# Folding the channel axis of a Fourier stage on Trainium2, with the first batch's Fourier part placed between the second batch's output products

## Chip, cores and metric

The kernel runs on one core of a Trainium2 chip. The metric is the device time of one execution in microseconds (us); TensorE is the matrix engine, VectorE, ScalarE and GpSimd are the elementwise engines, and SyncE issues all DMAs. In the profile they are called PE (its weight loads PEld), DVE, ACT, POOL and SP.

## What is computed

Three stages in float32, on 2 batches, 768 positions and 8 heads of 64 channels (512 channels together):

```python
# 1. attention among positions whose 6-bit hashes agree
scores = np.where(q_bucket == k_bucket, scale * q @ k.T, -1e9)
x = softmax(scores) @ v                      # (2, 768, 512)
# 2. gated projection
gate = sigmoid(causal_conv5(x, conv_w));  y = (gate * (x @ w_val)) @ w_out
# 3. Fourier mixing and a feed-forward block
mixed = np.real(np.fft.fft(np.fft.fft(y, axis=1), axis=2))
u = y + mixed
un = (u - mean(u)) / sqrt(var(u) + 1e-6)
out = u + relu(un @ w_ch1) @ w_ch2
```

## The kernel before

Every engine runs a program of its own, in the order in which it is written; semaphores tie them together. There is no scheduler: the order of calls in each engine's block is the order of work. TensorE takes float32 values that were rounded to a short form (fp32r), so nearly every operand is kept as a high and a low part, and one product (`product`, whose matmuls all carry line 1090) is three matmuls: high by high, low by high, high by low. ScalarE writes the high part, VectorE or GpSimd the low part (the value minus its high part).

- **Attention.** A software pipeline over 96 units (16 heads of 6 tiles). Before unit 0, SyncE loads the first two heads, the penalty column, then in its step -12 heads 2 and 3, the 128x128 identity (line 471), the values and the first weight chunks. VectorE converts the identity to bf16 (line 903) ahead of its first row maximum (`maximum`, line 830), since it is needed to turn the maxima.
- **Values and outputs.** `values(b, r)` forms x @ w_val for a half of a batch, in 4 banks of PSUM; VectorE multiplies it by the gate (`gate_values`, line 945), ScalarE rounds it (`hi_gv`), VectorE takes the rest (`lo_gv`, line 933). `outputs(b)` (line 1223) forms 6 tiles of y of 128 positions, each of 12 matmuls of 512 columns, and ScalarE copies them out of PSUM (`copy_y`). An output of the first 384 positions waits for the first 12 of the 16 low parts of the gated values, one of the last 384 for all 16.
- **Fourier part along the positions.** A sequence of 768 is folded: position s plus, and minus, position s+384 (`fold_tile`, line 950, 6 tiles of 128x512), which gives even and odd frequencies. `along_sequence(b)` (line 1237) has 8 groups, one for each 128 channels and parity, each of 9 matmuls with 386 or 384 columns (cosine and sine beside each other). ScalarE and VectorE split each result (`hi_seq`, `lo_seq`, lines 738 and 963).
- **Fourier part along the channels.** `along_channels(b, t)` (line 1253): for each of 6 tiles of positions, 4 blocks of 128 channels, cosine (258 columns) and sine (256), three matmuls each: 24 matmuls a tile. VectorE adds the result to y in four pieces and takes the tile's statistics (`add_mixed`, lines 972 to 980).
- **Feed-forward.** `hidden` and `project` run over 16 blocks of the hidden layer, for 4 blocks of 384 positions. Their weights are loaded through a staging buffer of two halves and split on the way: for w_1, GpSimd does chunks 0 to 9 alone (lines 529 and 597), and ScalarE (line 778) and GpSimd (line 608) share chunks 10 to 15; for w_2 GpSimd does all. ScalarE's calls alternate: two late chunks of w_1, then one tile of the turned normalised values (`hi_un`, line 751), three times; VectorE's low part of such a tile is `lo_un` (line 1020). TensorE starts `hidden(0, 0)` when all three `lo_un` are done.
- **Order.** TensorE: values and outputs of batch 0, of batch 1, then sequence and channels of batch 0, sequence and channels of batch 1, feed-forward. GpSimd: 16 chunks of the Fourier tables (`split_tables`), 6 low parts of folds (`lo_fold`, line 585), w_1 chunks 0 to 3, folds and low parts of batch 1, w_1 chunks 4 to 9, the late six, w_2.

## Time and profile before

| | before |
|---|---|
| time, median of 3 runs | 714.03 us (714.02 to 714.39) |
| time of the profiled execution | 714.04 us |
| its span, first to last instruction | 712.2 us |
| TensorE busy | 684.7 us, 96% of the span |
| VectorE, ScalarE, GpSimd busy | 388.9, 243.8, 203.0 us |
| mean granted clock of TensorE | 0.987 of full speed |
| chain that ended last | 92% TensorE, 3% VectorE, 1% DMA |

A busy share is an average over stages: the same TensorE can be without a gap in one stage and idle in the next. A row of the timeline gives the start in us from the span's start, the duration, the engine, the line, the operation, output and inputs, and in brackets how long the engine was idle before and what released it. Matmuls overlap, so the cost of one in a row of them is the distance between two starts, not its own duration.

### The profile page before, as it was taken

The numbers are of one execution on the slowest core, as the hardware profiler recorded it, in microseconds if no ns is written. First come the engines' busy times: TensorE is split into PE (matmuls) and PEld (weight loads), VectorE is DVE, ScalarE is ACT, GpSimd is POOL, SyncE is SP. The second block draws the span as 40 slices with busy tenths as digits, with TensorE's granted clock in tenths as the row PEclk, the third lists the DMA queues.
The fourth block names the chain that finished last, engine by engine and source line by source line (L and its number), as shares of the span: only waits on it lengthen the run. The fifth ranks groups of instructions, "written<-read, shape, count | busy, mean of one in ns | idle before, by whom it ended". The sixth has DMA issues, their size and how long they took to land.

```text
span 712.2 us, 10036 instructions
## 1 busy us (share of the span) xinstructions
PE 684.7 (96%) x3600; PEld 614.7 (86%) x3600; DVE 388.9 (55%) x621; ACT 243.8 (34%) x376; POOL 203.0 (29%) x193
## 2 busy tenths in 40 slices
PE   3699999999999999999999999999999999999998
PEld 2588888888888888798989999999999999999997
DVE  3566768888888888958745796321222122212112
ACT  2065545555555455654345241111112111211110
POOL 0001323232323233538848965880000000000000
PEclk9699999999999999999999999999999999999999
DMA  5945565555655441212202132330100010001001
GB/s 152 249 134 142 131 173 139 166 149 156 154 157 154 119 123 53 75 39 57 55 30 60 31 90 89 89 90 0 45 0 0 0 44 0 0 0 44 1 1 44
DMA packets 43846, 57.64 MB, mean 81 GB/s; under 512 B 21520, under 2 KB 25872, under 8 KB 43808
## 3 DMA queue, kind: packets, MB, share of 16 engines
q1 hardware_dynamic: 43808, 57.14, 29.0%
q8 instruction: 23, 0.38, 0.2%
q14 instruction: 15, 0.12, 0.1%
HBM read 31.81 MB, written 3.24 MB: 49 GB/s over the span
## 4 chain that ended last, share of the span: by engine, by line
PE 92%; DVE 3%; ACT 1%; DMA 1%; SPq 1%; issue 1%; DVEq 0%
PE psum L1090 74%; PE psum L1175 5%; PE psum L1176 4%; PE psum L1182 1%; PE psum L1183 1%; PE psum L1184 1%; PE psum L1187 1%; PE psum L1188 1%; PE psum L1185 1%; PE psum L1157 1%; DVE max_col L830 1%; PE psum L1278 1%; DMA ident<-in_ident_in 1%; DMA qk_raw<-in_qk 1%; ACT probs L669 1%
## 5 line engine op out<-in xcount | busy, mean ns | idle before, releaser
L1061 DVE SCALAR_TENSOR_TENSOR h_lo<-psum,h_hi 128x384 fp32r<-128x384 f32 x64 | 35.7, 558 | 184.2 <-ACT h_hi L791 184.2
L830 DVE TENSOR_REDUCE max_col<-psum 128x1 f32<-128x768 f32 x96 | 91.2, 953 | 40.8 <-PE psum L1090 40.6
L791 ACT ACTIVATE h_hi<-psum 128x384 fp32r<-128x384 f32 x64 | 31.5, 492 | 215.4 <-PE psum L1090 215.4
L669 ACT ACTIVATE probs<-psum 128x768 f32<-128x768 f32 x96 | 77.6, 809 | 39.8 <-PE psum L1090 39.8
L1090 PE MATMUL psum<-unt_hi,w_hi 128*128 (+1 forms) x256 | 86.9, 339 | 0.0
L1090 PE MATMUL psum<-unt_lo,w_hi 128*128 (+1 forms) x256 | 86.3, 337 | 0.0
L1090 PE MATMUL psum<-unt_hi,w_lo 128*128 (+1 forms) x256 | 85.9, 336 | 0.0
L1090 PE MATMUL psum<-a1k,a1q 128*128 128x384 f32 x192 | 67.9, 354 | 11.8 <-DVE max_col L830 6.7
L1090 PE MATMUL psum<-a1q,a1k 128*128 128x384 f32 x192 | 76.0, 396 | 0.8 <-ACT a2q L657 0.8
L1090 PE MATMUL psum<-w_lo,h_hi 128*128 128x512 f32 x192 | 75.9, 395 | 0.0
L1090 PE MATMUL psum<-w_hi,h_lo 128*128 128x512 f32 x192 | 75.8, 395 | 0.0
L1090 PE MATMUL psum<-w_hi,h_hi 128*128 128x512 f32 x192 | 74.6, 389 | 0.0
L1090 PE MATMUL psum<-a2k,a2q 96*128 96x384 f32 x192 | 67.2, 350 | 0.0
L546 POOL TENSOR_TENSOR vl<-v,vh 128x384 fp32r<-128x384 f32 x16 | 20.5, 1284 | 156.7 <-issue 81.6
L1090 PE MATMUL psum<-a2q,a2k 99*128 99x384 f32 x192 | 65.0, 339 | 0.0
L666 ACT ACTIVATE p_hi<-psum 128x768 fp32r<-128x768 f32 x48 | 39.0, 813 | 65.2 <-PE psum L1090 63.5
L836 DVE TENSOR_TENSOR p_lo<-probs,p_hi 128x768 fp32r<-128x768 f32 x48 | 54.0, 1125 | 3.2 <-ACT probs L669 3.2
L557 POOL TENSOR_TENSOR xT<-sums,rec_b 64x768 f32<-64x768 f32 x16 | 30.0, 1872 | 79.0 <-DMA rec_b<-rec_dram 74.4
L1090 PEld LDWEIGHTS psum<-unt_hi,w_hi 128*128 128x128 f32 x256 | 48.1, 188 | 2.2
L1090 PEld LDWEIGHTS psum<-unt_hi,w_lo 128*128 128x128 f32 x256 | 48.1, 188 | 2.2
L1090 PEld LDWEIGHTS psum<-a1k,a1q 128*128 128x128 f32 x192 | 38.2, 199 | 13.3 <-DVE max_col L830 7.3
L1090 PEld LDWEIGHTS psum<-unt_lo,w_hi 128*128 128x128 f32 x256 | 48.0, 188 | 0.0
(129 smaller groups left out, 1449.6 us busy)
## 6 DMA issues: line engine op xcount, KB each, us to landing
stg_w<-in_w SPq DMA_DIRECT2D x32, 256.0 KB, 2.6
qk_raw<-in_qk SPq DMA_DIRECT2D x16, 384.0 KB, 5.1
a1k<-qk_hi SPq DMA_DIRECT2D x32, 192.0 KB, 3.3
flag_b<-flag_dram SPq DMA_DIRECT2D x16, 384.0 KB, 4.2
a1q<-qk_hi SPq DMA_DIRECT2D x16, 192.0 KB, 2.8
a2q<-qk_hi SPq DMA_DIRECT2D x16, 192.0 KB, 3.5
a1q<-qk_lo SPq DMA_DIRECT2D x16, 192.0 KB, 3.7
a2k<-qk_lo SPq DMA_DIRECT2D x16, 192.0 KB, 3.7
```

The lines of the kernel that those rows point to most:

```text
L546: pool.tensor_tensor(vl[par][:, :].rearrange("p (t d) -> p t d", d=P), split_tiles(v1[par][:, :]), bits(vh[par][:, :]).rearrange("p (t d) ...
L557: pool.tensor_tensor(xT[rows, slot * S:(slot + 1) * S], sums[par][rows, :], rec_b[rows, :], ALU.mult).then_inc(x_ready, 1)
L666: act.activation(halves(p_hi[k % PHBUF][:, 0:S]), ring("st", i), ACT.Exp, scale=SCALE).then_inc(p_hi_ready, 1)
L669: act.activation(halves(probs[i % PBUF][:, 0:S]), ring("st", i), ACT.Exp, scale=SCALE).then_inc(probs_ready, 1)
L791: act.activation(h_hi[:, (j % 2) * HALF:(j % 2 + 1) * HALF], psum[:, j % 2, 0:HALF], ACT.Relu).then_inc(h_hi_ready, 1)
L830: dve.tensor_reduce(max_col[:, i % T:i % T + 1], ring("s", i), AX.XY, ALU.max).then_inc(max_done, 1)
L836: dve.tensor_tensor(p_lo[i % PBUF][:, 0:S], probs[i % PBUF][:, 0:S], bits(p_hi[k % PHBUF][:, 0:S]), ALU.subtract).then_inc(p_lo_ready, 1)
L1061: dve.scalar_tensor_tensor(h_lo[:, half], psum[:, j % 2, 0:HALF], 0.0, bits(h_hi[:, half]), ALU.max, ALU.subtract).then_inc(h_lo_ready, 1)
L1090: mm = pe.matmul(dst, lhs, rhs, start=first and n == 0, stop=last and n == len(pairs) - 1)
L1157: mm = pe.matmul(out_ps[0:MPARTS, t // HT, (t % HT) * P:(t % HT + 1) * P], neg_parts[:, MPARTS * t:MPARTS * (t + 1)], ident_b[:, :], start ...
L1175: pe.matmul(first, v1[par][:, w], probs[i % PBUF][:, 0:HALF], start=start, stop=stop)
L1176: pe.matmul(last, v1[par][:, w], probs[i % PBUF][:, HALF:PCOLS], start=start, stop=stop).then_inc(pv_done, 1)
```

## The change

- **The channel axis is folded too.** The real part of a transform over 512 channels needs channel c only together with channel 512-c: their sum meets the cosines, their difference the sines. So after the fold along the positions each tile is folded along the channels (`fold_tile`, now three VectorE instructions for one: the 512-column fold into `fold`, then a 256-column sum and a 256-column difference with the reversed half into `cf`). The sum goes only to the cosine columns and the difference only to the sine columns: `along_sequence` has 4 groups of 18 matmuls with 194 or 192 columns, and `along_channels` has 2 blocks in place of 4, 12 matmuls a tile.
- **Channel 0 has no partner.** It is carried apart: `fold_zero` (four tiny VectorE instructions), `zero_along_sequence` (12 matmuls with 2 weight columns and 194 or 192 moving ones), two small copies on ScalarE and two small subtractions on VectorE, and one more matmul a tile of `along_channels`, of 258 columns, against a row of ones. GpSimd fills that row and a tile of zeros before the tables.
- **The tables are shorter**: 16 chunks of 210 columns in place of 274.
- **The order.** Output tiles are made in the order 0, 3, 1, 4, 2, 5. TensorE does two outputs of batch 1, the whole sequence part of batch 0, then twice two tiles of its channel part and two outputs, then its last two tiles and the sequence part of batch 1. The folds of batch 0 move to VectorE's loop over the gated values of batch 1; those of batch 1 stand between the `add_mixed` of batch 0, all on VectorE. GpSimd's first four chunks of w_1 stand between its low parts of batch 1. VectorE's `inverse_deviations(0)` moves behind the split of batch 1, and the weights of the feed-forward get other addresses.
- **The identity** is loaded in SyncE's fifth DMA, and no longer in step -12.

The core of the diff:

```diff
-NE = HALF // 2 + 1
+NE = HALF // 2 + 2
 NO = HALF // 2
 EV, OD = 2 * NE, 2 * NO
+CM = CT // 2
+CH = C // 2
 NC_ = C // 2 + 2
 NS_ = C // 2
-WB_USED = HT * (EV + OD) + CT * (NC_ + NS_)
...
+WB_USED = HT * (EV + OD) + CM * (NC_ + NS_)
...
+Y_ORDER = (0, 3, 1, 4, 2, 5)
+FOLDS = (0, 3, 1, 4, 2, 5)
+NCF = 4
+SEQ = ((0, 0), (1, 0), (0, 1), (1, 1))
+SEQ_BANK = ((0, 1, 2, 3), (6, 4, 5, 7))
+ZERO_BANK = (6, 2)
+OUT_BANK = (4, 5, 7)
...
+        def channel_banks(b, t):
+            return 2 * (t % 3) if b else 2 * (t % 2)
...
             load_qk(1)
             sp.dma_start(pencol[:, :], pen_in).then_inc(pen_loaded, 16)
+            sp.dma_start(ident[:, :], ident_in).then_inc(ident_loaded, 16)
...
-                    sp.dma_start(ident[:, :], ident_in).then_inc(ident_loaded, 16)
...
+            def lo_fold(b, k):
+                n, f = T * b + k, FOLDS[k]
+                pool.wait_ge(cf_ready, 2 * (n + 1))
+                pool.wait_ge(f_hi_ready, n + 1)
+                if b > 0 and k == 0:
+                    pool.wait_ge(seq_done, len(SEQ) * b)
+                pool.tensor_tensor(f_lo[:, f * C:(f + 1) * C], cf[:, (n % NCF) * C:(n % NCF + 1) * C],
+                                   bits(f_hi[b][:, f * C:(f + 1) * C]), ALU.subtract).then_inc(f_lo_ready, 1)
...
+            pool.memset(bits(ones_row[:, :]), 1.0).then_inc(zeros_ready, 1)
+            pool.memset(bits(u0t[:, :]), 0.0).then_inc(zeros_ready, 1)
             split_tables((0, NH // 2))
-            lo_fold(0)
+            for k in range(T):
+                lo_fold(0, k)
+            pool.wait_ge(val_done, 2 * CT * B)
+            lo_fold(1, 0)
+            lo_fold(1, 1)
+            split_w1((0, W1_EARLY // 4))
+            lo_fold(1, 2)
+            lo_fold(1, 3)
+            split_w1((W1_EARLY // 4, W1_EARLY // 2))
+            lo_fold(1, 4)
+            lo_fold(1, 5)
             pool.wait_ge(y_done, B * T)
-            split_w1((0, W1_EARLY // 2))
-            fold_tile(1, 0)
-            pool.wait_ge(seq_done, 2 * CT)
-            lo_fold(1)
             split_w1((W1_EARLY // 2, (W1_N - W1_LATE) // 2))
+            pool.wait_ge(seq_done, len(SEQ) * B)
...
-            hi_gv(1)
-            for t in range(T):
-                copy_y(1, t)
-                if t < HT:
-                    hi_fold(0, 2 * t)
-                    hi_fold(0, 2 * t + 1)
-            hi_seq(0)
-            for f in range(T):
-                hi_fold(1, f)
+            for k in range(HT, T):
+                copy_y(0, k)
+            for i in range(2 * CT):
+                hi_gv(1, i)
+                if i < T:
+                    hi_fold(0, i)
+            copy_y(1, 0)
+            copy_y(1, 1)
+            hi_spectrum(0)
+            for k in range(2, T, 2):
+                hi_fold(1, k - 2)
+                hi_fold(1, k - 1)
+                copy_y(1, k)
+                copy_y(1, k + 1)
+            hi_fold(1, T - 2)
+            hi_fold(1, T - 1)
+            hi_spectrum(1)
             deviations(0)
-            hi_seq(1)
...
+            def fold_tile(b, k):
+                n, f = T * b + k, FOLDS[k]
                 kt, odd = f % HT, f // HT
+                base = n % 2 * C
+                dve.wait_ge(y_ready, T * b + 2 * (kt + 1))
+                dve.tensor_tensor(fold[:, base:base + C], y3[:, T * b + kt, :], y3[:, T * b + kt + HT, :],
+                                  ALU.subtract if odd else ALU.add).then_inc(fold_ready, 1)
+                dve.wait_ge(fold_ready, n + 1)
+                if n >= NCF:
+                    dve.wait_ge(f_lo_ready, n - NCF + 1)
+                up, down = fold[:, base + 1:base + CH + 1], fold[:, base + C - 1:base + CH - 1:-1]
+                dst = cf[:, n % NCF * C:(n % NCF + 1) * C]
+                dve.tensor_tensor(dst[:, 0:CH], up, down, ALU.add).then_inc(cf_ready, 1)
+                dve.tensor_tensor(dst[:, CH:C], up, down, ALU.subtract).then_inc(cf_ready, 1)
...
+            def fold_zero(b):
+                if b > 0:
+                    dve.wait_ge(y0_done, b)
                 dve.wait_ge(y_ready, T * (b + 1))
...
+                first, second = y3[:, T * b:T * b + HT, 0], y3[:, T * b + HT:T * (b + 1), 0]
+                dve.tensor_tensor(y0_raw[:, 0:HT], first, second, ALU.add).then_inc(y0_step, 1)
+                dve.tensor_tensor(y0_raw[:, HT:T], first, second, ALU.subtract).then_inc(y0_step, 1)
...
-            for r in range(2):
-                gate_values(1, r)
+            for i in range(2 * CT):
+                gate_value(1, i)
+                if i < T:
+                    fold_tile(0, i)
             lo_gv(4 * CT - 1)
-            for f in range(T):
-                fold_tile(0, f)
-            for n in range(2 * CT):
-                lo_seq(0, n)
-            for t in range(T):
-                add_mixed(0, t)
+            fold_zero(0)
+            fold_tile(1, 0)
+            lo_spectrum(0)
+            fold_tile(1, 1)
+            add_mixed(0, 0)
+            add_mixed(0, 1)
+            fold_tile(1, 2)
+            fold_tile(1, 3)
+            add_mixed(0, 2)
+            add_mixed(0, 3)
+            fold_tile(1, 4)
+            fold_tile(1, 5)
+            fold_zero(1)
+            add_mixed(0, 4)
+            add_mixed(0, 5)
             variances(0)
-            for n in range(2 * CT):
-                lo_seq(1, n)
-                if n == 0:
-                    inverse_deviations(0)
+            lo_spectrum(1)
+            inverse_deviations(0)
...
+            def output(b, k):
+                t = Y_ORDER[k]
+                pe.wait_ge(g_lo_ready, 2 * CT * b + CT * (t // HT + 1))
+                if b == 0:
+                    bank = 4 + k % 4
+                    if k >= 4:
+                        pe.wait_ge(y_ready, k - 3)
+                else:
+                    bank = OUT_BANK[k % 3]
+                    pe.wait_ge(y_ready, T * b + k - 2 if k >= 3 else T * b)
...
+            def along_sequence(b, k):
+                m, odd = SEQ[k]
+                n, base = (NO, WB_OD) if odd else (NE, WB_EV)
+                if k == 0:
+                    pe.wait_ge(gv_ready, 2 * CT * B)
+                    pe.wait_ge(y_ready, T * (b + 1))
+                pe.wait_ge(f_lo_ready, T * b + T - 1 + odd)
+                for a in range(2):
                     for kt in range(HT):
+                        at_ = (HT * odd + kt) * C + a * CH + m * P
+                        f, w = slice(at_, at_ + P), slice(base + (2 * kt + a) * n, base + (2 * kt + a + 1) * n)
+                        product(psum[:, SEQ_BANK[b][k], a * n:(a + 1) * n], three(f_hi[b][:, f], f_lo[:, f], wb_hi[:, w], wb_lo[:, w]),
+                                done=seq_done if a and kt == HT - 1 else None, first=kt == 0, last=kt == HT - 1)
+            def zero_along_sequence(b):
+                pe.wait_ge(y0_ready, b + 1)
+                if b > 0:
+                    pe.wait_ge(u_step, 4 * T * b)
+                for odd, n, base in ((0, NE, WB_EV), (1, NO, WB_OD)):
+                    for kt in range(HT):
+                        f, w = slice(2 * (HT * odd + kt), 2 * (HT * odd + kt + 1)), slice(base + 2 * kt * n, base + (2 * kt + 1) * n)
+                        product(psum[0:2, ZERO_BANK[b], odd * NE:odd * NE + n], [(y0_parts[:, f], wb_hi[:, w]), (y0_parts[:, f], wb_lo[:, w])],
+                                done=y0_done if odd and kt == HT - 1 else None, first=kt == 0, last=kt == HT - 1)
...
             def along_channels(b, t):
-                if T * b + t >= 3:
+                if b == 0 and t >= 2:
+                    pe.wait_ge(u_step, 4 * (t - 1))
+                if b > 0:
                     pe.wait_ge(u_step, 4 * (T * b + t - 2))
-                if t == 0:
-                    pe.wait_ge(seq_lo_ready, 4 * CT * b + 12)
-                for m in range(CT):
-                    if t == 0 and m == CT - 1:
-                        pe.wait_ge(seq_lo_ready, 4 * CT * b + 4 * (m + 1))
+                bank = channel_banks(b, t)
+                for m in range(CM):
+                    if t == 0:
+                        pe.wait_ge(seq_lo_ready, 2 * (len(SEQ) * b + 3 + m))
                     for a, base, cols in ((0, WB_COS, NC_), (1, WB_SIN, NS_)):
                         f = slice((2 * m + a) * S + t * P, (2 * m + a) * S + (t + 1) * P)
                         w = slice(base + m * cols, base + (m + 1) * cols)
-                        product(psum[:, 2 * (t % 3) + a, 0:cols], three(pq_t_hi[:, f], pq_t_lo[:, f], wb_hi[:, w], wb_lo[:, w]),
-                                done=ch_done if a and m == CT - 1 else None, first=m == 0, last=m == CT - 1)
+                        product(psum[:, bank + a, 0:cols], three(pq_t_hi[:, f], pq_t_lo[:, f], wb_hi[:, w], wb_lo[:, w]),
+                                first=m == 0, last=a == 1 and m == CM - 1)
+                if t == 0:
+                    pe.wait_ge(u0_lo_ready, 2 * (b + 1))
+                pe.matmul(psum[:, bank, 0:NC_], u0t[0:D, t * P:(t + 1) * P], ones_row[0:D, :], start=False, stop=True).then_inc(ch_done, 1)
...
-            outputs(0)
+            for k in range(T):
+                output(0, k)
             values(1, 0)
             values(1, 1)
-            outputs(1)
-            pe.wait_ge(gv_ready, 2 * CT * B)
+            output(1, 0)
+            output(1, 1)
             pe.wait_ge(wb_split, -(-WB_COS // WB_CH))
-            along_sequence(0)
+            spectra(0)
             pe.wait_ge(wb_split, NH)
-            pe.wait_ge(y_ready, B * T)
-            for t in range(T):
-                along_channels(0, t)
-            along_sequence(1)
+            pe.wait_ge(zeros_ready, 2)
+            along_channels(0, 0)
+            along_channels(0, 1)
+            output(1, 2)
+            output(1, 3)
+            along_channels(0, 2)
+            along_channels(0, 3)
+            output(1, 4)
+            output(1, 5)
+            along_channels(0, 4)
+            along_channels(0, 5)
+            spectra(1)
...
+    c = np.arange(1, CH + 1)[:, None]
+    cos = np.cos(2 * np.pi * ((c * np.arange(NC_)[None, :]) % C) / C)
+    cos[CH - 1] *= 0.5
+    cos = cos.reshape(CM, P, -1)
+    sin = np.sin(2 * np.pi * ((c * np.arange(NS_)[None, :]) % C) / C).reshape(CM, P, -1)```

VectorE, from the first gated value of batch 1 to the end of its folds (gv is the gated value, g_lo its low part, fold and cf the folds). Before:

```order
L945 TENSOR_TENSOR gv<-gate,psum 128x384 x2
L933 TENSOR_TENSOR g_lo<-gv,g_hi 128x384
L945 TENSOR_TENSOR gv<-gate,psum 128x384
L933 TENSOR_TENSOR g_lo<-gv,g_hi 128x384
...
L933 TENSOR_TENSOR g_lo<-gv,g_hi 128x384 x2
L956 TENSOR_TENSOR fold<-y 128x512 x6
L963 TENSOR_TENSOR pq_t_lo<-psum,pq_t_hi 128x2x192 x16
```

With the change:

```order
L1003 TENSOR_TENSOR gv<-gate,psum 128x384
L991 TENSOR_TENSOR g_lo<-gv,g_hi 128x384
L1014 TENSOR_TENSOR fold<-y 128x512
L1021 TENSOR_TENSOR cf<-fold 128x256
L1022 TENSOR_TENSOR cf<-fold 128x256
...
L1003 TENSOR_TENSOR gv<-gate,psum 128x384
L991 TENSOR_TENSOR g_lo<-gv,g_hi 128x384 x2
L1030 TENSOR_TENSOR y_raw<-y 128x3
```

Three fold instructions now stand behind each of the first six gated values, ahead of the low parts for which the outputs wait.

GpSimd, from the tables to the late chunks of w_1 (rows of a loop stand once). Before:

```order
L585 TENSOR_TENSOR f_lo<-fold,f_hi 128x512 x6
L590 UNCONDITIONAL_BRANCH
...
L575 TENSOR_TENSOR fold<-y 128x512 x2
L585 TENSOR_TENSOR f_lo<-fold,f_hi 128x512
L575 TENSOR_TENSOR fold<-y 128x512
...
L608 TENSOR_TENSOR w_lo<-stg_w,w_hi 128x512 x6
```

With the change:

```order
L611 TENSOR_TENSOR f_lo<-cf,f_hi_129 128x512 x6
L611 TENSOR_TENSOR f_lo<-cf,f_hi_130 128x512 x2
...
L564 TENSOR_TENSOR w_hi<-stg_w,ones 128x512
L623 TENSOR_TENSOR w_lo<-stg_w,w_hi 128x512
...
L611 TENSOR_TENSOR f_lo<-cf,f_hi_130 128x512 x2
...
L634 TENSOR_TENSOR w_lo<-stg_w,w_hi 128x512 x6
```

GpSimd's six folds of batch 1 are gone, and its low parts of batch 1 stand in pairs with two chunks of w_1 behind each of the first two pairs.

## Rows read from the trace of the kernel before

**Rows 1.** The page; then one stretch: length, busy PE, PEld, DVE, ACT, POOL, clock.

```profile
PE 684.7 (96%) x3600; PEld 614.7 (86%) x3600; DVE 388.9 (55%) x621; ACT 243.8 (34%) x376; POOL 203.0 (29%) x193
...
374.30:441.40 67.10, 66.06 (x470) 65.51 (x469) 49.92 (x111) 25.58 (x51) 49.71 (x42) 1.00 0.22 64
```

**Rows 2.** The chain that ended last, in the first 45 us (start, us, what); then ScalarE.

```profile
21.48 4.62 DMA ident<-in_ident_in
...
28.09 0.87 DVE qk_lo L814
...
24.77 0.83 ACT L639 CAST qk_hi<-qk_raw 128x768 fp32r<-128x768 f32 x1 [11.18 <-DMA qk_raw<-in_qk]
```

**Rows 3.** TensorE's timeline: 512, 386, 258 columns; weight loads of four transposes; float32 pair.

```profile
357.94 0.39 PE L1090 MATMUL psum<-wa_hi,g_hi 128*128 128x512 f32 x1
...
374.30 0.33 PE L1090 MATMUL psum<-wb_hi,f_hi 128*128 128x386 f32 x1
...
374.65 0.34 PE L1090 MATMUL psum<-wb_lo,f_hi 128*128 128x386 f32 x1
...
387.02 0.28 PE L1090 MATMUL psum<-wb_hi,pq_t_hi 128*128 128x258 f32 x1
387.14 0.28 PE L1090 MATMUL psum<-wb_hi,pq_t_lo 128*128 128x258 f32 x1
...
424.31 0.47 PEld L1278 LDWEIGHTS psum<-ident,un 128*128 128x128 f32 x4
424.74 0.19 PEld L1090 LDWEIGHTS psum<-wb_hi,pq_t_hi 128*128 128x128 f32 x1
...
42.87 0.65 PE psum L1175 x2
```

**Rows 4.** TensorE's timeline after a long wait near the start.

```profile
27.27 0.69 PE L1090 MATMUL psum<-a1k,a1q 128*128 128x384 f32 x1 [6.66 <-DVE max_col L830]
...
31.32 0.52 PE L1090 MATMUL psum<-a1k,a1q 128*128 128x384 f32 x1
31.64 0.40 PE L1090 MATMUL psum<-a2k,a2q 96*128 96x384 f32 x1
```

**Rows 5.** VectorE's timeline: last gated value, last low part, first folds of batch 0.

```profile
358.14 0.55 DVE L945 TENSOR_TENSOR gv<-gate,psum 128x384 f32<-128x384 f32 x1 [1.06 <-PE psum L1090]
...
359.34 0.56 DVE L933 TENSOR_TENSOR g_lo<-gv,g_hi 128x384 fp32r<-128x384 f32 x1 [0.18 <-ACT g_hi L715]
359.81 1.29 DVE L956 TENSOR_TENSOR fold<-y 128x512 f32<-128x512 f32 x2
```

**Rows 6.** VectorE's next two folds, and GpSimd's low parts of folds at that time.

```profile
363.55 2.30 DVE L956 TENSOR_TENSOR fold<-y 128x512 f32<-128x512 f32 x2 [2.44 <-POOL f_lo L585]
...
362.15 2.54 POOL L585 TENSOR_TENSOR f_lo<-fold,f_hi 128x512 fp32r<-128x512 f32 x2 [6.43 <-ACT f_hi L729]
```

**Rows 7.** GpSimd's timeline: the end of the tables; chunks of w_1; the last late ones.

```profile
354.84 0.88 POOL L597 TENSOR_TENSOR wb_lo<-stg_b,wb_hi 128x274 f32 x1 [0.17 <-POOL wb_hi L529]
...
401.74 1.05 POOL L529 TENSOR_TENSOR w_hi<-stg_w,ones 128x512 f32 x1
...
416.64 1.30 POOL L597 TENSOR_TENSOR w_lo<-stg_w,w_hi 128x512 f32 x1 [0.26 <-POOL w_hi L529]
...
430.95 2.70 POOL L608 TENSOR_TENSOR w_lo<-stg_w,w_hi 128x512 fp32r<-128x512 f32 x2 [2.17 <-ACT w_hi L778]
```

**Rows 8.** VectorE: low parts of the last sequence group; first piece of two `add_mixed`.

```profile
388.16 1.02 DVE L963 TENSOR_TENSOR pq_t_lo<-psum,pq_t_hi 128x384 fp32r<-128x384 f32 x2 [0.58 <-ACT pq_t_hi L738]
...
422.62 0.41 DVE L972 TENSOR_TENSOR y<-y,psum 128x257 f32<-128x257 f32 x1
...
424.80 0.41 DVE L972 TENSOR_TENSOR y<-y,psum 128x257 f32<-128x257 f32 x1
```

**Rows 9.** TensorE's first output product of the feed-forward; the page's row on the w loads.

```profile
441.37 0.39 PE L1090 MATMUL psum<-w_hi,h_hi 128*128 128x512 f32 x1
...
stg_w<-in_w SPq DMA_DIRECT2D x32, 256.0 KB, 2.6
```

250 lines of the change are left out of this document (131 added, 119 removed).

## The prediction

> **What bounds the kernel now.** I read the page first: TensorE is busy for 684.7 of the 712.2 us of the span, the other engines for 55% at most [rows 1]. Next I read the engines stage by stage, because a change of the Fourier part is worth what TensorE's queue is worth there. From the first sequence matmul of batch 0 to the first output product of the feed-forward, TensorE is busy for 66.06 of 67.10 us, VectorE for 49.92 and GpSimd for 49.71 [rows 1]. So matmuls set the time there, but the next two engines have only 17 us to spare. Last I read the chain at the start: the identity, issued at 21.48, holds VectorE until 26.1 [rows 2]. The sum below is made against the profiled execution, 714.04 us, of which 712.2 are span; the median of the runs is 714.03, so nothing has to be carried over. A difference of 0.2% (1.4 us) is about what can be told from none.
>
> **The matmuls that go.** A matmul costs the distance between two starts: 0.12 us at 258 columns, 0.175 at 386 (two steps in 0.35), 0.228 at 512 (72 of them between 357.94 and 374.30) [rows 3].
> - Channels: 12 fewer in each of 12 tiles, 144 x 0.12 = 17.3 us less.
> - Sequence: 144 stay, with half the columns. No row has such a matmul. The lower bound is the straight line through 258 and 386 columns, 0.055 us for 128 columns, which gives 0.091 at 193. The upper one is 0.12: it should not cost more than one of 258 columns. Four transposes, which load 128 weight columns each and move only 128, took 0.43 us by the starts of their weight loads, 0.107 each [rows 3]. I take 0.108, since the weights are as wide here: 144 x (0.175 - 0.108) = 9.7 us less (8 to 12).
> - Added: 24 matmuls with two weight columns at 0.09, 2.2 us, and 12 against the row of ones, 1.4 us.
>
> Together 17.3 + 9.7 - 2.2 - 1.4 = 23.4 us of TensorE's queue. The Trainium skill ("TensorE: Matmul & The Clock Gate", section on the back-to-back issue gap) gives a stream of weight loads and matmuls about 81 ns at 128 columns and 131 at 512. The trace disagrees at 512, with 0.228 us. By that page 193 columns would cost an estimated 0.09 us, and 2.6 us more would go.
>
> **The start.** Without the identity VectorE takes its first two maxima while it waits for head 2. It goes on with qk_lo when ScalarE's qk_hi is there, at 24.77 + 0.83 = 25.6, and not at 28.09: 2.5 us less [rows 2]. The bounds are 1.5 and 2.5, since TensorE may still be at its low clock when the next hash comes; I take 2.2. The DMA that is put in front (0.4 us of SyncE) stands in a pause of that queue, and costs nothing.
>
> **The folds in VectorE's loop.** Here I expect the gain to be lost. Before, the last low part of the gated values is done at 359.9 [rows 5], and TensorE needs it at 357.94 + 12 x 0.228 = 360.7 for its second output of batch 1, which is now of the last 384 positions. Now six folds stand in front of it:
> - Own time: a fold is 0.65 us (two in 1.29) [rows 5]; I put the two half-width ones at 0.33 each and the wait between at 0.1, so 1.4 us, six times 8.4 us. The eight value groups of batch 1, 12 x 0.175 each, end at 357.94, so the first is complete at about 343.4. From there the loop needs 8 x 0.48 for gated values, 8 x 0.47 for low parts and 8.4 for folds: 359.4. That alone would still fit.
> - Lock: two folds that started while GpSimd ran took 2.30 us where two cost 1.29. The first began at 363.55 and must have stood until GpSimd's operation ended at 364.69 [rows 6]. VectorE with both operands in SBUF and GpSimd exclude each other; a multiplication with PSUM (0.55 at 358.14) does not suffer [rows 5]. In the loop 4 of VectorE's 5 operations are of that kind. GpSimd is still at the tables (its last ends at 355.7 [rows 7]; now some 2 us earlier, being shorter, behind two fills of 1.1 us), and then at once at six low parts of folds, each with about 1.2 us of lock. I lay the two queues beside each other, each waiting for what the other has begun: 3.5 us lost to the tables, 6.5 to the six low parts.
>
> That makes 359.4 + 10 + 0.4 = 369.8 for the last low part (bounds: 360.7 if no operation meets another, 372 if all do). Low part 12, needed at 357.94, comes at about 360.3. TensorE waits 2.3 us, makes one output, waits 6.8. After a wait of 6.66 us its matmuls of 384 columns stood 0.32 us apart, the 1.2 GHz level, from 27.27 to 31.64 [rows 4], against 0.175 at 2.4 GHz: such a wait costs another 2.0 us. The second output ends at 369.9 + 2.7 + 2.0 = 374.6, where before all six ended at 374.3.
>
> **From there to the last output of batch 1.** Sequence part: 72 x 0.108 + 12 x 0.09 = 8.9. Wait for the last group's split: before, it came 2.15 us after the end of the group (387.02 to 389.18 [rows 3, 8]), hidden by three of the four channel blocks; now only one block of 0.7 covers it: 1.5. Four channel tiles of 13 x 0.12, 6.2, and four outputs, 10.9. The end is at 402.1, before it was at 374.3: **27.8 later**.
>
> **From there to the first output product of the feed-forward**: 67.1 us before (441.37 [rows 9] less 374.3). TensorE now has 3.1 + 8.9 + 9.4 for channels, sequence and channels, 1.3 for transposes, 4.2 for two hidden blocks, 26.9 in all, but it will not be the bound. GpSimd's queue is: the last two folds wait for the last y, meet two more chunks of w_1 and each other (copy 0.7, two folds with lock waits 3.4, high part 0.6, low parts and the rest 3.7: 8.4 us). Then six chunks of w_1 at the pace of before (401.74 to 417.94, 16.2 us [rows 7]). Then the six late ones, bound by the two halves of the buffer: load 2.8, round 0.6, low part 1.3 for each half in turn, 14.1 us in all (before 15.7, to 433.65 [rows 7]). Only then is the last `lo_un` done: 402.1 + 8.4 + 16.2 + 14.1 = 440.8. TensorE starts its hidden blocks there, again after 5 us of waiting and so at 1.2 GHz: 4.2 + 2.0. The first chunk of w_2 asks 2.6 for the load [rows 9] and 2.4 for the split, 446.2, and is covered. The product starts at **447.0**, 44.9 behind the last output: 22.2 less. VectorE's six `add_mixed` of 2.18 us [rows 8] fill the same stretch and end at about 445.
>
> **Sum.** 27.8 - 22.2 = 5.6 later in this stage, 2.2 earlier at the start: 714.0 + 3.4 = **717.4 us**. Behind that TensorE's rows are the same. The case's own range is 712 to 722.
>
> **Rivals.**
> - **The locks meet seldom.** The low parts are ready at 360.7, and TensorE does not wait at its outputs. Then all behind moves by 9.1 of waiting and 2.0 of clock: 717.4 - 11.1 = 706 us. It speaks for it that GpSimd waits for DMAs between its tables, and that in the old loop eight low parts lost only about 1 us; against it, that VectorE's queue is now full. It is decided at 369.8: each us earlier gives one back, and below 366 the result turns to faster. Chance 0.3.
> - **TensorE stays the bound throughout.** 714.0 - 23.4 - 2.2 = 688 us. It needs GpSimd's w_1 work to be hidden, which the 38.7 us from last y to last late chunk deny. 0.05.
> - **The tail is longer.** The late chunks take 15.7 as before, every short wait of TensorE lowers its clock, and GpSimd's locks also hold the tiny instructions of channel 0 and of the deviations: 5 us more, 722. 0.15.
> - **Short fp32r matmuls cost like float32 ones.** A float32 product of 384 columns takes two records of 0.325 us [rows 3], 1.69 ns a column, so 0.33 at 193: 144 x 0.22 = 32 us more, 749 us. 0.05.
>
> **How the numbers follow.** The forecast has 0.45. The predicted time is its 717.4. Below 702 lie TensorE as the bound and a part of the first rival, above 724 the short matmuls and a part of the long tail, together 2 in 10: range 702 to 724. Faster takes the first two rivals and 0.03 of the forecast: 0.38. Same, 712.6 to 715.5, is 0.1 out of the forecast. Slower has the rest: 0.52.
>
> **What would show it.** On VectorE, folds of 1.1 to 1.9 us beside GpSimd's low parts, and the last g_lo near 368 (2 us earlier than above, for the start). On TensorE, a wait of about 7 us for g_lo with a granted clock of 0.5 behind it; sequence matmuls 0.108 us apart; small waits for pq_t_lo; a last wait for unt_lo of about 5 us. On GpSimd, w_1 without a pause from the last y on. I am wrong at the first step if TensorE has no gap at its second output of batch 1, at the last if unt_lo waits for VectorE and not for the late chunks.

## The result, and the profile after

| | before | changed |
|---|---|---|
| median | 714.25 us (5 runs, 714.02 to 714.64) | 719.07 us (5 runs, 718.08 to 721.08) |
| ratio, 95% interval | | 1.0073 [1.0053, 1.0093] |
| profiled execution | 714.04 us, span 712.2 | 720.74 us, span 719.0 |

The changed kernel is slower by 0.7%. Its profiled execution lies 1.7 us above its median, so the two traces differ by 6.7 us and the medians by 4.8. The page of the changed kernel, and two pieces of the stretch that answers to [rows 1] (length, busy PE, PEld, DVE, ACT, POOL, clock):

```profile
PE 675.1 (94%) x3492; PEld 600.0 (83%) x3492; DVE 400.7 (56%) x647; ACT 238.2 (33%) x364; POOL 193.1 (27%) x189
...
358.00:375.00 17.00, 10.30 (x48) 8.51 (x49) 11.39 (x22) 4.99 (x10) 3.82 (x3) 0.80 0.10 32
...
405.00:445.00 40.00, 29.96 (x190) 27.01 (x189) 32.20 (x76) 12.44 (x23) 25.61 (x22) 0.85 0.29 86
```

The work of TensorE went, and its waiting came: before it was busy for 66.06 of 67.10 us, now it is for 10.30 of 17 us and for 29.96 of 40, at a mean granted clock of 0.80 and 0.85. What it waited for from 340 to 450 (us in total, times, longest one); before, this view had one row, one wait of 1.0 us for pq_t_lo:

```profile
PE psum L1193 <- DVE g_lo L991: 7.2, 2, 5.8
PE psum L1193 <- DVE y L1066: 3.6, 1, 3.6
PE psum L1406 <- DVE unt_lo L1114: 2.5, 1, 2.5
PE psum L1193 <- DVE pq_t_lo L1042: 2.1, 3, 1.0
PE psum L1193 <- POOL f_lo L611: 1.8, 1, 1.8
PE psum L1193 <- DVE y L1072: 1.1, 2, 0.8
```

TensorE's timeline, where [rows 3] and [rows 9] have their like: second output of batch 1, first matmuls of the spectra, those with two weight columns, the row of ones, the end of the last output, the feed-forward.

```profile
358.88 0.50 PE L1193 MATMUL psum<-wa_hi,g_hi 128*128 128x512 f32 x1 [1.35 <-DVE g_lo L991]
...
367.71 0.80 PE L1193 MATMUL psum<-wa_hi,g_hi 128*128 128x512 f32 x1 [5.81 <-DVE g_lo L991]
...
372.43 0.25 PE L1193 MATMUL psum<-wb_hi,f_hi 128*128 128x194 f32 x1
...
376.43 0.25 PE L1193 MATMUL psum<-wb_hi,y_parts 128*2 128x194 f32 x1
...
377.49 0.27 PE L1193 MATMUL psum<-wb_hi,f_hi 128*128 128x192 f32 x1
...
386.34 0.28 PE L1193 MATMUL psum<-wb_lo,pq_t_hi 128*128 128x256 f32 x1
386.55 0.38 PE L1394 MATMUL psum<-ones_row,u0t 64*128 64x258 f32 x1
386.86 0.50 PE L1193 MATMUL psum<-wa_hi,g_hi 128*128 128x512 f32 x1
387.19 0.40 PE L1193 MATMUL psum<-wa_hi,g_lo 128*128 128x512 f32 x1
...
401.80 0.28 PE L1193 MATMUL psum<-wb_hi,pq_t_hi 128*128 128x258 f32 x1
...
441.20 0.68 PE L1193 MATMUL psum<-unt_hi,w_hi 128*128 x1 [3.63 <-DVE y L1066]
...
448.07 0.39 PE L1193 MATMUL psum<-w_hi,h_hi 128*128 128x512 f32 x1
```

The reader is to see four things. Between 372.43 and 376.43 stand 36 short matmuls, 0.111 us each, and the twelve with two weight columns take 0.088. The output that begins at 367.71 takes 4.72 us, where 12 x 0.228 is 2.7: after the wait of 5.81 its first nine matmuls stood 0.43 us apart, which is the 1.2 GHz level, and only the rest 0.23. The last output ends at 401.80, 27.5 us later than before (374.30). From there to the first product it is 46.3 us (before 67.1). The rest of the kernel takes 270.9 us and took 270.8.

VectorE at the end of the gated-value loop (compare [rows 5]), and GpSimd at that time and behind the last y (compare [rows 7]):

```profile
358.75 1.77 DVE L1014 TENSOR_TENSOR fold<-y 128x512 f32<-128x512 f32 x1
360.56 0.42 DVE L1021 TENSOR_TENSOR cf<-fold 128x256 f32<-128x256 f32 x1
...
361.23 0.55 DVE L1003 TENSOR_TENSOR gv<-gate,psum 128x384 f32<-128x384 f32 x1
...
366.25 1.41 DVE L991 TENSOR_TENSOR g_lo<-gv,g_hi 128x384 fp32r<-128x384 f32 x2
```

```profile
358.69 1.29 POOL L611 TENSOR_TENSOR f_lo<-cf,f_hi 128x512 fp32r<-128x512 f32 x1 [1.41 <-ACT f_hi L761]
...
409.56 1.05 POOL L564 TENSOR_TENSOR w_hi<-stg_w,ones 128x512 f32 x1
...
424.51 1.27 POOL L623 TENSOR_TENSOR w_lo<-stg_w,w_hi 128x512 f32 x1 [0.17 <-POOL w_hi L564]
...
439.65 1.27 POOL L634 TENSOR_TENSOR w_lo<-stg_w,w_hi 128x512 fp32r<-128x512 f32 x1 [2.19 <-ACT w_hi L836]
```

The fold at 358.75 takes 1.77 and not 0.65: GpSimd's low part ran from 358.69 to 359.98. The last low part of the gated values ends at 367.66. GpSimd begins the last six early chunks of w_1 at 409.56, 7.8 us behind the last output, needs 16.2 us for them and 15.1 for the six late ones.

The end of that stage, on ScalarE and then on VectorE:

```profile
438.95 0.62 ACT L836 CAST w_hi<-stg_w 128x512 fp32r<-128x512 f32 x1 [2.97 <-DMA stg_w<-in_w]
439.48 0.58 ACT L802 CAST unt_hi<-psum 128x512 fp32r<-128x512 f32 x1
...
440.09 0.69 DVE L1114 TENSOR_TENSOR unt_lo<-psum,unt_hi 128x512 fp32r<-128x512 f32 x1 [1.85 <-ACT unt_hi L802]
```

ScalarE waits for the load of the last late chunk, whose half of the buffer GpSimd had to empty first. The last high part of the normalised values (unt_hi) stands behind that chunk, and VectorE's low part (unt_lo) waits for it. TensorE starts its feed-forward at 441.20, 0.4 us behind the end of unt_lo. Its row names a piece of y as what released it, but the program waits there for unt_lo; the tiles of y that it also waits for were done at 437.5.

### The profile page after: what moved, and what is told of

It reads as the page before. It is cut to its first block, busy times and chain, and to the rows that moved or that the text cites. A ratio compares the mean times of both kernels' runs of the same rounds, so it can differ in the third digit from the quotient of the medians.

```text
span 719.0 us, 9813 instructions
## 1 busy us (share of the span) xinstructions
PE 675.1 (94%) x3492; PEld 600.0 (83%) x3492; DVE 400.7 (56%) x647; ACT 238.2 (33%) x364; POOL 193.1 (27%) x189
## 4 chain that ended last, share of the span: by engine, by line
PE 85%; DVE 5%; DMA 3%; issue 2%; ACT 2%; POOL 2%; SPq 1%; POOLq 0%; DVEq 0%
PE psum L1193 67%; PE psum L1278 5%; PE psum L1279 4%; DMA stg_w<-in_w 2%; DVE fold L1014 1%; PE psum L1285 1%; PE psum L1286 1%; DMA qk_raw<-in_qk 1%; PE psum L1287 1%; PE psum L1290 1%; PE psum L1291 1%; PE psum L1288 1%; PE psum L1260 1%; DVE cf L1022 1%; POOL w_lo L623 1%
## 5 line engine op out<-in xcount | busy, mean ns | idle before, releaser
L1193 PE MATMUL psum<-unt_hi,w_hi 128*128 (+1 forms) x256 | 88.2, 344 | 3.6 <-DVE y L1066 3.6
L1193 PE MATMUL psum<-unt_lo,w_hi 128*128 (+1 forms) x256 | 87.3, 341 | 0.0
L1193 PE MATMUL psum<-unt_hi,w_lo 128*128 (+1 forms) x256 | 87.0, 340 | 0.0
L1193 PE MATMUL psum<-a1k,a1q 128*128 128x384 f32 x192 | 67.1, 350 | 10.5 <-DVE max_col L888 5.5
L1193 PE MATMUL psum<-a1q,a1k 128*128 128x384 f32 x192 | 76.0, 396 | 0.8 <-ACT a2q L692 0.8
L1193 PE MATMUL psum<-w_lo,h_hi 128*128 128x512 f32 x192 | 75.9, 395 | 0.0
L1193 PE MATMUL psum<-w_hi,h_lo 128*128 128x512 f32 x192 | 75.8, 395 | 0.0
L1193 PE MATMUL psum<-w_hi,h_hi 128*128 128x512 f32 x192 | 74.6, 389 | 0.0
L1193 PE MATMUL psum<-a2k,a2q 96*128 96x384 f32 x192 | 66.4, 346 | 0.0
L1193 PE MATMUL psum<-a2q,a2k 99*128 99x384 f32 x192 | 65.1, 339 | 0.0
L1193 PEld LDWEIGHTS psum<-unt_hi,w_hi 128*128 128x128 f32 x256 | 49.0, 191 | 6.1 <-issue 3.8
L1193 PEld LDWEIGHTS psum<-unt_hi,w_lo 128*128 128x128 f32 x256 | 48.9, 191 | 2.2
L1193 PEld LDWEIGHTS psum<-unt_lo,w_hi 128*128 128x128 f32 x256 | 48.9, 191 | 0.0
L1193 PEld LDWEIGHTS psum<-a1k,a1q 128*128 128x128 f32 x192 | 37.7, 197 | 11.8 <-DVE max_col L888 5.8
## 6 DMA issues: line engine op xcount, KB each, us to landing
stg_w<-in_w SPq DMA_DIRECT2D x32, 256.0 KB, 2.6
```

Source lines behind the costliest of these rows:

```text
L1193: mm = pe.matmul(dst, lhs, rhs, start=first and n == 0, stop=last and n == len(pairs) - 1)
```

## The experiments

All times are medians of 4 to 11 runs beside runs of the kernel before on the same chip (medians 714.05 to 714.26 us). The trace is of one run, which can lie up to 3 us off the median. The diffs are against the changed kernel if nothing else is said.

**1. The identity alone, and the change without it.** In the kernel before, and in the changed one the other way round:

```diff
             sp.dma_start(pencol[:, :], pen_in).then_inc(pen_loaded, 16)
+            sp.dma_start(ident[:, :], ident_in).then_inc(ident_loaded, 16)
...
-                    sp.dma_start(ident[:, :], ident_in).then_inc(ident_loaded, 16)
```

> The kernel before, with nothing changed but the place of the identity's load (behind the penalty column instead of behind heads 2 and 3). If the start is worth what the forecast took (VectorE no longer stands for the identity, the low part of head 2 comes at 25.6 instead of 28.09), the time falls by 2.2 us, from 714.2 to 712.0. If the changed kernel's trace tells it right (its first high part of the probabilities comes only 0.8 us earlier, because something else is late next), the time falls by 0.7 us, to 713.5, and TensorE waits for head 2 or for a maximum longer than the forecast had.

> The changed kernel with the identity's load where it was before. If the start gains in the changed kernel what it gained alone (712.4 against 714.05, 1.7 us), the time is 720.8, 1.7 more than the changed kernel's 719.1; by the profiled start of the changed kernel (0.7 to 0.8 us earlier) it is 719.8.

Measured: 712.38 us, 0.9979 of before [0.997, 0.9987], 1.7 us less; and 721.25 us, 1.0096 [1.008, 1.0111], which is 2.2 more than the changed kernel by the medians and 1.6 by the ratios. So the start is worth 1.7 us in the kernel before. In the changed one it looks like as much, but the two intervals overlap. One trace cannot size it: ScalarE's first p_hi came at 40.3 before, at 39.9 with the identity late, and between 38.0 and 39.6 in the twelve traces with the identity in front. The changed kernel's, 39.6, is among the latest.

**2. Folds behind the loop.** VectorE and ScalarE only:

```diff
             for i in range(2 * CT):
                 gate_value(1, i)
-                if i < T:
-                    fold_tile(0, i)
             lo_gv(4 * CT - 1)
+            for k in range(T):
+                fold_tile(0, k)
```

> The changed kernel, with batch 0's six folds taken out of VectorE's gated-value loop and put behind the last low part; the order on TensorE stays. If the folds in the loop (own time and locks) are what holds g_lo, TensorE's 5.8 us wait for g_lo at its second output of batch 1 goes, and that output ends near 363.5 instead of 372.4; but the last low fold then comes near 370 (six folds of 1.4 us behind 358.9, and 2.5 us to the low part), so the wait turns up again as one for f_lo of about 6 us, with TensorE at 1.2 GHz behind it: 717 us, 2 less than the changed kernel's 719.1. If only the lock with the table splits costs, folds behind the tables run at 1.3 us and the wait for f_lo is 4 us or less: 715 us. If the outputs' late start had another cause than VectorE's queue (the tables, GpSimd), the wait for g_lo stays: 719 us.

Measured: 723.08 us, 1.0122 [1.0103, 1.0141]: 4 us more than the changed kernel, where all my theories had less or the same. The wait for g_lo is gone, so the folds in the loop were its cause. But the wait turns up again as one for f_lo, of 9.92 us and not of the 6 expected. The profiled execution took 720.09 us, 3 less than the median and no more than that of the changed kernel (720.74), so the trace does not show where the 4 us lie. It shows what held f_lo: behind the loop a fold does not run at its own 1.4 us. VectorE, then GpSimd, then TensorE of this kernel:

```profile
362.78 0.42 DVE L1023 TENSOR_TENSOR cf<-fold 128x256 f32<-128x256 f32 x1
363.12 1.48 DVE L1024 TENSOR_TENSOR cf<-fold 128x256 f32<-128x256 f32 x1
364.53 0.68 DVE L1016 TENSOR_TENSOR fold<-y 128x512 f32<-128x512 f32 x1
```

```profile
362.94 1.38 POOL L611 TENSOR_TENSOR f_lo<-cf,f_hi 128x512 fp32r<-128x512 f32 x1 [1.08 <-ACT f_hi L761]
```

```profile
371.86 0.50 PE L1195 MATMUL psum<-wb_hi,f_hi 128*128 128x194 f32 x1 [9.92 <-POOL f_lo L611]
```

The two queues fall into step: each fold's last operation starts while GpSimd makes the low part of the fold before, and stands until that ends (362.94 + 1.38 = 364.32; it ends at 364.60). The first fold takes 1.40 us, the second 2.50 and the other four 2.46 or 2.47. In the loop some low parts fall beside multiplications with PSUM, which do not stand.

**3. Folds behind, four outputs as cover.** As 2, and on TensorE (ScalarE's copies follow the same order):

```diff
-            output(1, 0)
-            output(1, 1)
+            for k in range(4):
+                output(1, k)
...
             along_channels(0, 1)
-            output(1, 2)
-            output(1, 3)
+            output(1, 4)
+            output(1, 5)
             along_channels(0, 2)
             along_channels(0, 3)
-            output(1, 4)
-            output(1, 5)
```

> As the kernel with the folds behind, and TensorE also makes the third and fourth output of batch 1 ahead of the first spectra (the last two stand behind the first two channel tiles). The folds then have four outputs (10.9 us) as cover. By the forecast's account no wait for g_lo or f_lo over 1.5 us is left and the last output of batch 1 ends near 390 (changed kernel 401.8). What GpSimd has to do behind it (low folds, six chunks of w_1 in 16.2 us, six late ones in 15.1) keeps its length but starts later than the last y, since two pairs of early chunks still stand in its queue: unt_lo near 430 instead of 440.8, and 708.5 us in all. If VectorE's queue and not GpSimd's is the bound there, the first product of the feed-forward moves by no more than 4 us: 715 us. If TensorE is the bound, all 12 us are gained: 707 or less.

Measured: 718.84 us, 1.0077 [1.0064, 1.009]. Waits for f_lo of 4.5 us before batch 0's spectra and 4.2 before batch 1's. From the second on the folds again took 2.46 to 2.50 us each, which I had priced at 1.4.

**4. The chunks of w_1 in another order.** Chunks 8 to 11, whose places nobody uses any more, are split first, in GpSimd's idle time before batch 1's folds; of the others four early ones are left behind the last y, and four late ones (the chunks lie in that order in DRAM, and the feed-forward waits for twelve at once):

```diff
+W1_ORDER = [8, 9, 10, 11, 0, 1, 2, 3, 4, 5, 6, 7, 12, 13, 14, 15]
...
+            split_w1((0, 2), first=-8)
             lo_fold(1, 0)
             lo_fold(1, 1)
-            split_w1((0, W1_EARLY // 4))
+            split_w1((2, 3), first=4)
...
-            split_w1((W1_EARLY // 2, (W1_N - W1_LATE) // 2))
+            split_w1((4, 6), first=4)
```

> The changed kernel, with the 16 chunks of w_1 split in another order: chunks 8 to 11, whose places are free as soon as the values are done, first, in GpSimd's idle time before the second batch's folds; four instead of six are then left for GpSimd behind the last y, and four instead of six late ones with ScalarE. If the forecast's last step is right (the feed-forward starts when GpSimd's queue of w_1 is through), the late ones end about 10 us earlier, and the next thing late is VectorE: add_mixed and low parts from 424.6 on, which end at 439.7 instead of 445.1, so that the first product comes near 440 instead of 448.1: 711 us (709 to 713). If VectorE, or TensorE's own clock, is the bound there already, the feed-forward starts less than 2 us earlier: 717 to 719 us.

Measured: 711.81 us, 0.9962 [0.9949, 0.9975], 7.3 less than the changed kernel. In its trace (714.70 us, the slowest of its six runs) the last late chunk ends at 429.8 instead of 440.9, and the feed-forward starts at 436.21 instead of 441.20. So GpSimd's queue of w_1 was the bound at the end of the stage. The next one is VectorE, as expected: its last unt_lo (435.11 to 435.78) has no idle time ahead of it.

**5. VectorE makes the low parts of the folds itself**, on top of 4; GpSimd then splits w_1 as soon as the places are free:

```diff
-                pool.tensor_tensor(f_lo[:, f * C:(f + 1) * C], cf[:, (n % NCF) * C:(n % NCF + 1) * C],
+                dve.tensor_tensor(f_lo[:, f * C:(f + 1) * C], cf[:, (n % NCF) * C:(n % NCF + 1) * C],
...
             split_w1((0, 2), first=-8)
-            lo_fold(1, 0)
...
+            pool.wait_ge(seq_done, len(SEQ))
+            split_w1((2, 4), first=4)
```

> As the kernel with the other order of w_1, and the twelve low parts of the folds are made by VectorE itself (0.65 us each) and not by GpSimd (1.28 each). Lock theory: in the runs so far a fold whose predecessor's low part runs on GpSimd takes VectorE 2.46 us instead of 1.4, so the 0.65 of its own is cheaper than the 1.06 of standing. The last g_lo comes near 365.5 instead of 367.7, the wait of TensorE for it is 3.5 us instead of 5.8; GpSimd begins the middle four chunks of w_1 at the last y (about 400) and not 7.5 us behind it: 708 us against 711.8. Rival, VectorE's own work is what counts and the lock is small: 12 x 0.65 = 7.8 us are added to VectorE's queue, the wait for g_lo grows, and the time is 715 or more.

Measured: 717.35 us, 1.0034 [1.0021, 1.0047], 5.5 more than 4. In the loop it held in part: the folds run at their own time once the tables are through, but the wait for g_lo is 5.12 us where I expected 3.5. Behind the last y it did not: VectorE's two folds now meet the chunks of w_1 and last from 401.56 to 409.70, 8.1 us, and TensorE waits 6.80 us for f_lo:

```profile
405.40 1.77 DVE L998 TENSOR_TENSOR fold<-y 128x512 f32<-128x512 f32 x1
407.21 1.15 DVE L1005 TENSOR_TENSOR cf<-fold 128x256 f32<-128x256 f32 x1
408.28 1.50 DVE L1006 TENSOR_TENSOR cf<-fold 128x256 f32<-128x256 f32 x1
```

The rival's price was right, by a cause that neither theory had: not the low parts, but who runs beside the folds. Experiment 9 keeps the low parts on VectorE and is the fastest of all.

**6. Three outputs first**, on top of 5. VectorE's order follows: the second fold of batch 1 now stands ahead of the split of the first spectra (`lo_spectrum`), and the other folds and low parts stand in pairs.

```diff
-Y_ORDER = (0, 3, 1, 4, 2, 5)
+Y_ORDER = (0, 1, 3, 4, 2, 5)
...
-            output(1, 0)
-            output(1, 1)
+            for k in range(HT):
+                output(1, k)
...
             along_channels(0, 1)
...
+            for k in range(HT, T):
+                output(1, k)
```

> As the kernel with VectorE's own low parts, and TensorE makes three outputs of batch 1 first, the first two of the first half (tiles 0, 1, 3), so that the last g_lo is needed 2.7 us later and the folds have 2.7 us more cover; the other three outputs stand together behind the first two channel tiles. By the account of VectorE's queue: no wait for g_lo over 0.5 us, first spectra near 366 instead of 372.4, last output near 388 instead of 402; from there VectorE is the bound (some 56 us of folds, low parts, additions and norms behind 364), the feed-forward starts near 426 to 430: 701 us (699 to 705). If instead the stage is bound by GpSimd's w_1 even now, nothing but the first 6 us is gained: 706. If waits for channel tiles' additions (y) appear and lower TensorE's clock: 706 to 710.

Measured: 717.14 us, 1.0043 [1.0027, 1.0058]. I had expected 701. The spectra begin at 367.86, but TensorE then waits 3.5 us for pq_t_lo and 6.7 for y: the first two folds of batch 1 last from 368.68 to 376.39, the last two from 394.98 to 403.12, beside w_1 again. The second of these folds, and GpSimd, which begins 0.04 us ahead of it:

```profile
372.03 1.80 DVE L1000 TENSOR_TENSOR fold<-y 128x512 f32<-128x512 f32 x1
...
371.99 1.29 POOL L614 TENSOR_TENSOR w_lo<-stg_w,w_hi 128x512 f32 x1 [0.17 <-POOL w_hi L565]
```

**7. All outputs of batch 1 ahead of the spectra**, as the kernel before had them. ScalarE's copies follow, and VectorE's third to sixth fold of batch 1 now alternate with the `add_mixed` and no longer stand in pairs; on TensorE:

```diff
-            output(1, 0)
-            output(1, 1)
+            for k in range(T):
+                output(1, k)
```

> The changed kernel with all six outputs of batch 1 ahead of batch 0's spectra, as the kernel before had it; folds, chunks of w_1 and the rest as in the changed kernel. It tells the fold along the channels from the new order. If GpSimd's queue sets the start of the feed-forward, it can do the second batch's low folds only after the first spectra, now near 392 instead of 381; low folds, four early chunks and locks then end near 413 and the ten others (16.2 + 15.1 us) near 444: 722 us, 3 more than the changed kernel. If the interleaving is what costs (the last y 27.7 us later than before), the time falls to 714 or less, as the last y then comes 18 us earlier.

Measured: 726.12 us, 1.0164 [1.0151, 1.0177], 7 more than the changed kernel. GpSimd can begin batch 1's low parts only at 394.32, and its last late chunk ends at 448.96. So the interleaving was not what cost: with the order on VectorE that goes with it, it gave 7 us. That is 4 more than expected. VectorE's folds, now beside w_1, also hold TensorE's channel tiles (8.1 us for y); how much of that comes from their new places, no run tells.

**8. Four folds in the loop**, on top of 4 (low parts on GpSimd), three outputs first as in 6:

```diff
-                if i < T:
+                if i < 4:
                     fold_tile(0, i)
             lo_gv(4 * CT - 1)
+            for k in range(4, T):
+                fold_tile(0, k)
...
             along_channels(0, 1)
-            output(1, 2)
             output(1, 3)
+            output(1, 4)
             along_channels(0, 2)
+            output(1, 5)
             along_channels(0, 3)
-            output(1, 4)
-            output(1, 5)
```

> As the kernel with the other order of w_1 (711.8 us; low parts on GpSimd again), with VectorE's queue made to fit: only four of batch 0's folds stay in the gated-value loop, the other two come behind the last low part; TensorE makes three outputs of batch 1 first (tiles 0, 1, 3), then the spectra, two channel tiles, two outputs, a channel tile, the last output, three channel tiles. By the account of VectorE's queue with 2.46 us for a fold whose predecessor's low part is on GpSimd: the last g_lo comes near 359, before it is needed at 362.6; the last f_lo near 365, when the third output ends; so the first spectra begin near 366 and not 372.4, with no lowered clock ahead. All behind is 6 to 9 us earlier, the last output near 391: 704 us (701 to 707). If what is gained ahead is lost to waits for VectorE's additions behind (VectorE's work from there is the same), the time stays above 709.

Measured: 713.0 us, 0.9989 [0.998, 0.9998]. I had expected 704. The spectra begin at 365.82, as expected, and yet it gains nothing over 4 (711.81): TensorE gives it back in one wait for VectorE, whose folds of batch 1 meet low parts and chunks of w_1.

```profile
402.73 0.58 PE L1202 MATMUL psum<-wb_hi,pq_t_hi 128*128 128x258 f32 x1 [8.18 <-DVE y L1079]
```

**9. GpSimd kept out of the folds.** As 6, with two waits of GpSimd and batch 0's sixth fold behind the last g_lo (against kernel 6):

```diff
             pool.wait_ge(val_done, 2 * CT * B)
+            pool.wait_ge(cf_ready, 2 * (T + 2))
             split_w1((0, 2), first=-8)
             pool.wait_ge(seq_done, len(SEQ))
-            split_w1((2, 4), first=4)
+            split_w1((2, 3), first=4)
+            pool.wait_ge(f_lo_ready, B * T)
             pool.wait_ge(y_done, B * T)
+            split_w1((3, 4), first=4)
```

> As the kernel with three outputs first and VectorE's own low parts (717.1 us), with GpSimd's chunks of w_1 kept out of the stretches in which VectorE works on folds: the first four wait for the second fold of batch 1, the last six early ones for that batch's last low part; and batch 0's sixth fold stands behind the last g_lo. No work is removed, none added but two waits of GpSimd. If it is the lock between VectorE's operations on two SBUF operands and GpSimd's that fills VectorE's queue (in the kernel with three outputs first, the folds of batch 1 and their first low parts took 11 us more than their own time), the feed-forward starts near 427 instead of 437.7: 707 us (704 to 710), and the folds of batch 1 run at 1.4 us each. If those long operations were not a matter of the lock, but of VectorE's own, delaying GpSimd gains nothing or makes the last chunks of w_1 late: 717 us or more.

Measured: **708.55 us**, 0.9936 [0.992, 0.9952], 8.6 less than 6, and below both kernels. The same first two folds of batch 1, and TensorE's first matmul of the feed-forward:

```profile
366.11 0.69 DVE L1005 TENSOR_TENSOR fold<-y 128x512 f32<-128x512 f32 x1 [0.90 <-ACT y L742]
366.84 0.43 DVE L1012 TENSOR_TENSOR cf<-fold 128x256 f32<-128x256 f32 x1
367.18 0.42 DVE L1013 TENSOR_TENSOR cf<-fold 128x256 f32<-128x256 f32 x1
367.52 0.69 DVE L1005 TENSOR_TENSOR fold<-y 128x512 f32<-128x512 f32 x1
368.24 0.42 DVE L1012 TENSOR_TENSOR cf<-fold 128x256 f32<-128x256 f32 x1
368.58 0.42 DVE L1013 TENSOR_TENSOR cf<-fold 128x256 f32<-128x256 f32 x1
```

```profile
429.99 0.44 PE L1204 MATMUL psum<-unt_hi,w_hi 128*128 x1 [1.54 <-DVE y L1067]
```

2.8 us for two folds, where kernel 6 had 7.7. The work of both engines is the same and GpSimd only waits more, so these 4.9 us are the price of running beside GpSimd. In the traces the feed-forward starts 7.75 us earlier than in kernel 6; 1.2 of that lie ahead of the stage (first gated value at 341.1, not 342.3), and the moved fold took the wait for g_lo from 2.0 to 0.6. I had expected 427 and not 430 for the feed-forward. Two waits of 2.80 us for y remain, and VectorE is still the bound. They come after a place where GpSimd still works beside VectorE's operations: there two low parts take 2.77 us (the last pair of the same kernel: 1.28) and the first operation of a fold 1.78 (alone 0.69).

**10. Channel 0 over 128 rows**, in the changed kernel and in kernel 9:

```diff
-                pe.matmul(psum[:, bank, 0:NC_], u0t[0:D, t * P:(t + 1) * P], ones_row[0:D, :], start=False, stop=True).then_inc(ch_done, 1)
+                pe.matmul(psum[:, bank, 0:NC_], u0t[:, t * P:(t + 1) * P], ones_row[:, :], start=False, stop=True).then_inc(ch_done, 1)
```

> The changed kernel, with the product of channel 0 against the row of ones made over all 128 rows instead of 64 (the other rows hold zeros). In the changed kernel's trace a channel tile takes 1.92 us from start to start (384.94 to 386.86) where 13 x 0.12 would be 1.56, and the gaps lie around the matmul of 64 rows: 0.21 ahead of it, 0.31 behind it, and 0.1 more at the next one. If it is the change of the number of rows that costs, it stands 0.12 from its neighbours now, the tile takes 1.56 to 1.6, and the last output of batch 1 ends 1.6 us earlier; the chain of GpSimd behind it moves with it: 717.5 us against 719.1. If the gap comes from something else (the wait at the end of the tile, the signal), it stays, and so does the time.

> The kernel in which GpSimd is kept out of the folds (708.55 us), with the same edit of channel 0's product. There VectorE is the bound behind the first spectra, so most of the 12 x 0.4 us are not on the path: 707.5 us (706.5 to 708.6). If TensorE's queue decides there, 704 us.

Measured: 717.82 us, 1.0053 [1.0039, 1.0067], 1.25 less than the changed kernel, though the intervals overlap; and 709.69 us, 0.9937 [0.9924, 0.9951], the same ratio as kernel 9, where I had expected 707.5. TensorE's timeline of the first:

```profile
385.52 0.28 PE L1193 MATMUL psum<-wb_lo,pq_t_hi 128*128 128x256 f32 x1
385.64 0.28 PE L1394 MATMUL psum<-ones_row,u0t 128*128 128x258 f32 x1
385.76 0.40 PE L1193 MATMUL psum<-wa_hi,g_hi 128*128 128x512 f32 x1
386.00 0.40 PE L1193 MATMUL psum<-wa_hi,g_lo 128*128 128x512 f32 x1
```

The gaps around the matmul are gone, and a tile takes 1.53 us instead of 1.92. In the changed kernel the last output ends at 399.78 and no longer at 401.80; 0.4 of that lies ahead (first gated value at 342.63, not 343.01), so 1.6 us are the tiles, as expected. In kernel 9, where VectorE is the bound, the time does not fall.

## Why the prediction was right, and where it was not

The direction came out, and the size lies in the range: 719.07 us against 717.4. The two engines that the forecast named as bounds, VectorE at the gated values and GpSimd at w_1, are the ones that TensorE waits for. By its steps, in the two traces, where the start is measured at TensorE's first value matmul of batch 1 (before, then changed):

```profile
341.27 0.33 PE L1090 MATMUL psum<-x_hi,wa_hi 128*128 128x384 f32 x1
...
340.70 0.33 PE L1193 MATMUL psum<-x_hi,wa_hi 128*128 128x384 f32 x1
```

| step | forecast | measured |
|---|---|---|
| start | -2.2 | -0.6 |
| last output of batch 1, behind the start | +27.8 | +28.1 |
| from there to the feed-forward's first product | -22.2 | -20.8 |
| together | +3.4 | +6.7 (medians: +4.8) |

The second row fits so well by luck. The second output of batch 1 ended 1.6 us earlier than forecast (372.43, against 374.6 less the 0.6 of the start), and from there to the last output it took 29.4 us and not 27.5.

- **Matmuls.** 0.111 us for 193 columns (forecast 0.108), 0.088 for two weight columns (0.09). The rival of short matmuls at float32's price is out. The term that failed is "12 against the row of ones, 1.4 us": a channel tile takes 1.92 us (384.94 to 386.86) and not 13 x 0.12, 1.56. Experiment 10 shows why: the matmul of 64 rows costs 0.4 us more than one of 128, the 0.1 at the next matmul included. That is 1.5 us in the four tiles of the second row. With the measured prices the saving of TensorE's queue is an estimated 17.3 + 9.2 - 2.1 - 6.0 = 18.4 us, and not 23.4.
- **Folds in the loop.** From VectorE's first gated value to the last g_lo the forecast had 26.4 us (343.4 to 369.8), and it took 24.7 (343.01 to 367.66). By the forecast's own times without a lock, 16.0 us, 8.7 were lost and not 10.4: 3.1 in the three folds beside the tables (3.5), the rest beside the low parts (6.5). The waits for g_lo are 1.35 and 5.81 us (2.3 and 6.8), and the low clock costs 2.0 us more (2.0). Experiment 2 took the folds out and the wait went. The rival in which the locks meet seldom is out.
- **The last step.** GpSimd's queue from the last output on: 7.8 + 16.2 + 15.1 us (8.4 + 16.2 + 14.1; the late chunks came between the forecast and the rival with the longer tail). Then 0.3 us until TensorE starts, and 6.87 for two hidden blocks (6.2), since it ran at the 1.2 GHz level from 441.20 to 446.8 (0.32 us from start to start). Experiment 4 shortened this queue and gained 7.3 us; experiment 7 made it start later and lost 7.
- **Start.** The cause was right: VectorE's qk_lo starts at 25.86 and no longer at 28.00 (forecast 25.6). The size was not: 2.2 us was taken near the upper bound of 1.5 to 2.5. Experiment 1 has 1.7, and in the changed kernel's trace TensorE is only 0.6 earlier, and as much with the identity late (340.71). What else is late at the start there stays open.
- **What it did not say.** I took the wait for g_lo as a loss that leaving the loop would give back. My expectations of experiments 2, 3, 5, 6 and 8 were 6 to 16 us too low. Their traces point to one reason: what a fold costs depends on what GpSimd does beside it, and once TensorE is fed earlier, VectorE's queue becomes the bound. The forecast priced the lock in the loop and at the last two folds, and I did not price it again where the new orders put the folds.

What stays open: where the 4 us of experiment 2 lie, how much of kernel 9's gain is the moved fold, and how far a schedule without the two last waits of 2.80 us would go.
